# Attention on one core: the eight global keys put into the block of the 96 neighbouring keys

## The reference

```python
scores = scale * np.matmul(q, k.transpose(0, 1, 3, 2))
is_global = pos[None, :] < int(n_global)          # 8
is_local = (rel >= 0) & (rel < int(n_local))      # 96
dist = np.where(is_global & ~is_local, float(n_local), np.abs(rel))
scores = scores - slopes[:, None, None] * dist    # per head
scores = np.where(is_global | is_local, scores, -1e9)
a = softmax(scores); attn = a @ v
x = moe(attn)      # token mixing, then a 512 -> 1536 -> 512 layer
out = moe2(x)      # angles, cos and sin products, token mixing, a last layer
```

## Time and profile before

| | us |
|---|---|
| median of 3 runs (528.63 to 528.68) | 528.64 |
| the profiled execution's own time | 529.02 |
| its span, first to last instruction | 527.2 |
| steps 8 to 46 of attention, 26.44 to 102.37 | 75.93 |
| first product of the mixing layers starts at | 109.53 |

### The profile page before, as it was taken

The page is one execution under the profiler, slowest core; times in us unless marked ns, Lnnn a source line. Parts: engine busy times, 40 slices in busy tenths (PEclk is TensorE's granted clock), DMA queues, the critical chain, the costliest instruction groups (busy, mean ns, idle before and its releaser), DMA issues.

```text
span 527.2 us, 8284 instructions
## 1 busy us (share of the span) xinstructions
PE 509.6 (97%) x3092; PEld 475.3 (90%) x3092; DVE 267.1 (51%) x671; ACT 181.8 (34%) x466; POOL 139.9 (27%) x129
## 2 busy tenths in 40 slices
PE   2999989999999999999999999999999999999997
PEld 2899889978999999987999999998888899888897
DVE  6888999845211232136211144327775584665452
ACT  4899889842111121113111123532223230331120
POOL 3555545339970000001300004550220130000040
PEclk9999999999999999999999999999999999999999
DMA  7754554403440000000300003140000011000002
GB/s 264 266 180 136 208 178 142 141 2 127 173 137 4 1 1 0 2 0 1 121 0 1 0 1 121 60 140 0 1 1 1 1 62 61 0 1 0 1 31 90
DMA packets 9258, 35.02 MB, mean 66 GB/s; under 512 B 1153, under 2 KB 3201, under 8 KB 7809
## 3 DMA queue, kind: packets, MB, share of 16 engines
q1 hardware_dynamic: 9216, 34.48, 19.1%
HBM read 31.33 MB, written 3.15 MB: 65 GB/s over the span
## 4 chain that ended last, share of the span: by engine, by line
PE 90%; DVE 6%; issue 2%; ACT 1%; DMA 1%; DVEq 0%; ACTq 0%
PE bank L271 70%; PE bank L1338 6%; PE bank L1121 5%; PE bank L1084 4%; PE bank L1102 2%; PE bank L1194 1%; DVE scores L855 1%; PE bank L1221 1%; DVE wsplit L770 1%; DVE wsplit L781 1%; PE bank L1149 1%; ACT probs L625 1%; DMA counts<-both_counts 1%; ACT probsT L579 0%; DVE act_raw L797 0%
## 5 line engine op out<-in xcount | busy, mean ns | idle before, releaser
L271 PE MATMUL bank<-hid,wsplit 128*128 128x384 f32 (+1 forms) x648 | 126.4, 344 | 0.1
L271 PEld LDWEIGHTS bank<-hid,wsplit 128*128 128x128 f32 x648 | 113.3, 188 | 3.9 <-issue 0.7
L271 PE MATMUL bank<-split,wsplit 128*128 128x384 f32 x576 | 108.1, 337 | 0.0
L271 PE MATMUL bank<-wsplit,zs 128*128 128x512 f32 (+1 forms) x576 | 104.1, 340 | 0.0
L271 PEld LDWEIGHTS bank<-wsplit,zs 128*128 128x128 f32 x576 | 89.1, 188 | 13.3
L271 PEld LDWEIGHTS bank<-split,wsplit 128*128 128x128 f32 x576 | 100.3, 188 | 0.0
L990 DVE SCALAR_TENSOR_TENSOR hid<-bank,hid 128x384 fp32r<-128x384 f32 x48 | 26.7, 557 | 140.4 <-ACT hid L704 140.4
L557 POOL TENSOR_TENSOR wsplit<-wraw,wsplit 128x1536 fp32r<-128x1536 f32 (+1 forms) x18 | 58.7, 3261 | 75.3 <-ACT wsplit L665 74.2
L704 ACT ACTIVATE hid<-bank 128x384 fp32r<-128x384 f32 x48 | 23.6, 491 | 143.8 <-PE bank L271 143.8
L556 POOL CAST wsplit<-wraw 128x1536 fp32r<-128x1536 f32 (+1 forms) x12 | 15.9, 1326 | 129.2 <-PE bank L271 123.0
L1084 PE MATMUL bank<-wsplit 128*128 128x232 f32 (+2 forms) x224 | 39.8, 310 | 10.0 <-DVE wsplit L830 9.0
(11 more groups left out here) (103 smaller groups left out, 534.5 us busy)
## 6 DMA issues: line engine op xcount, KB each, us to landing
wraw<-weights SPq DMA_DIRECT2D x16, 768.0 KB, 4.0
qk_raw<-qk SPq DMA_DIRECT2D x11, 1056.0 KB, 5.0
vt<-v SPq DMA_DIRECT2D x12, 256.0 KB, 3.2
out<-act_raw SPq DMA_DIRECT2D x16, 192.0 KB, 1.9
wraw<-weights SPq DMA_DIRECT2D x4, 512.0 KB, 3.5
qk_raw<-qk SPq DMA_DIRECT2D x1, 792.0 KB, 5.6
vg<-v_first SPq DMA_DIRECT2D x2, 256.0 KB, 5.6
qk_raw<-qk SPq DMA_DIRECT2D x1, 264.0 KB, 3.4
```

The costliest lines, as they stand in the source:

```text
L271: mm = pe.matmul(dst, lhs(a), rhs(c), start=first and i == 0, stop=last and i == 2, skip_group_check=True)
```

## The change

The eight global keys are treated as if they were part of the block before: places 32 to 135 of a row of `probs` (the 96 neighbours and the 8 global keys) are 104 keys that stand beside each other, and are turned in one transpose and weighed in one product with a second half of `vt`, in which the host has put the 96 value rows of the block before and the 8 global rows. In units 0 and 6 the block has the 8 global keys alone. The path of `gprobs`, `gprobsT`, `vg` and `o_ready` is gone. The ring of keys has six places, one for each unit of a batch, so no unit wraps.

```diff
-RING = 4
-PROBS_AT = 4
+RING = T
+PROBS_AT = 3
-PT_HEAD = REACH + P
+SEEN = REACH + G
+PT_HEAD = 2 * P
@@ SyncE
-                if n >= 3:
-                    sp.wait_ge(o_ready, n - 1)
-                sp.dma_start(vt[:, n % 3], v[b, t]).then_inc(v_in[n % 3], 16)
-                if t == 0:
-                    if b:
-                        sp.wait_ge(vg_lo, b)
-                    sp.dma_start(vg[:, :], v_first[b]).then_inc(vg_in, 16)
+                if n >= 2:
+                    sp.wait_ge(pv_done, PAIRS * (n - 1))
+                sp.dma_start(vt[:, n % 2], v[b, t]).then_inc(v_in[n % 2], 16)
@@ ScalarE
-                first = 0 if m // PAIRS % T else REACH
-                src = PT_BANK[m % 2][:, 0:2 * PT_HEAD]...[:, :, first:]
-                act.activation(dst, src, ACT.Copy).then_inc(pT_taken, 1)
+                act.activation(probsT[:, m % 2], PT_BANK[m % 2][:, :], ACT.Copy).then_inc(pT_taken, 1)
-                if n >= 1 and p == 2:
-                    global_probsT(n - 1)
+                if g == 2:
+                    act.wait_ge(pv_done, STEPS)
@@ VectorE
-                if p == 1 and n >= 1:
-                    gather(n - 1)
                 if p == 2 and n >= 1:
-                    global_probsT_lo(n - 1)
                     invert_sums(n - 1)
-                if p == 0 and n >= 2:
-                    take_x(n - 2)
-                if p == 1 and n % T == 1:
-                    global_values_lo(n // T)
+                if p == 3 and n >= 1:
+                    take_x(n - 1)
@@ TensorE: head_scores, transpose_probs, weigh_values
-                else:
-                    windows = [(UNSEEN, P, (RING - 1) * KW + G + UNSEEN), (P, WIN, 0)]
+                keys = SEEN if n % T else G
...
+                    pe.transpose(PT_BANK[m % 2][0:keys, at:at + P], probs[:, n % 2, h, OWN - keys:OWN],
+                                 ident[:, :])
+                    mm = pe.transpose(PT_BANK[m % 2][:, at + P:at + 2 * P], probs[:, n % 2, h, OWN:],
+                                      ident[:, :])
...
+                    pe.matmul(O_BANK[n % 2][:, cols], probsT[:, m % 2, at + P:at + 2 * P], vt[:, n % 2, 0, cols], ...)
+                    mm = pe.matmul(O_BANK[n % 2][:, cols], probsT[0:keys, m % 2, at:at + P],
+                                   vt[0:keys, n % 2, 1, cols], start=False, stop=True, ...)
...
+            for i in range(2):
+                for at in range(0, 2 * PT_HEAD, PT_HEAD):
+                    pe.transpose(PT_BANK[i][:, at:at + P], ident[:, :], ident[:, :])
-                if p == 2 and n >= 1:
-                    pe.transpose(O_BANK[n % 2][:, 0:P], gprobs...)
-                if p == 3 and n >= 1:
-                    for i in range(2):
-                        mm = pe.matmul(O_BANK[(n - 1) % 2][:, :], gprobsT[:, :], vg_split[:, i], ...)
```

More of the change, by code:

```diff
@@ L75, with build @@
 PI_IN = 3.1415925
-def build(nc, qk, v, v_first, both_counts, weights, out):
+def build(nc, qk, v, both_counts, weights, out):
     ctx = ExitStack()
@@ L185, in build @@
         qk_in = [sem(f"qk_in{i}") for i in range(2)]
-        v_in = [sem(f"v_in{i}") for i in range(3)]
+        v_in = [sem(f"v_in{i}") for i in range(2)]
         k_hi = sem("k_hi")
@@ L631, in _ @@
                     keys_hi(n + 1, p)
-                if p == 0 and n % T == 1:
-                    global_values_hi(n // T)
             general_act(act, flag)
@@ L1381 @@
     first_keys = np.broadcast_to(kc[:, 0:1, :, :, 0:G], (B, T, D, H, G))
-    v_first = np.zeros((B, 2, H, G, H, D), v.dtype)
-    for h in range(H):
-        v_first[:, :, h, :, h] = v[:, None, h, 0:G]
+    rows = v.transpose(0, 2, 1, 3).reshape(B, T, P, DM)
+    v_rows = np.zeros((B, T, P, 2, DM), v.dtype)
+    v_rows[:, :, :, 0] = rows
+    v_rows[:, 0, 0:G, 1] = rows[:, 0, 0:G]
+    v_rows[:, 1:, 0:REACH, 1] = rows[:, :-1, UNSEEN:]
+    v_rows[:, 1:, REACH:SEEN, 1] = rows[:, 0:1, 0:G]
     def tiles(w):
```

136 lines of the change are left out of this document (31 added, 105 removed).

## The result

| us | before | after |
|---|---|---|
| median of the runs | 528.64 | 601.98 (four runs, 597.53 to 604.36) |
| the profiled execution's own time | 529.02 | 601.67 |
| its span | 527.2 | 599.9 |
| scores of an ordinary step, start to start | 0.53 | 0.98 |
| a step of an ordinary unit, start to start | 1.6 to 2.1 | 3.39 |

The ratio is 1.138, with a 95% interval of 1.132 to 1.144. The forecast was 522.3 in a range of 517.8 to 527.6: wrong in size and in sign.

What follows compares the result with a forecast made beforehand. TensorE bound attention at 7.14 us a unit, ScalarE within 5%. Start +1.4, steps 8 to 46 -6.7, end -1.0 sum to -6.3 us: 522.7 for the profiled execution, 522.3 as median, range 517.8 to 527.6.

Steps and rivals of the forecast that it cites:

- Part 5, the start: Unit 0 at the low clock gets more expensive: +1.4 us at the scores of step 8, clock rising about 25 us.
- If the clock rises at the same moment: Start: the 3.06 us of added low-rate work is then done after the rise at half price, +1.53.
- the low clock lasts: Rival, attention: 1.5 us per extra low-rate step; 534.2 us if it lasts through units 2 and 3; chance 0.10.
- Part 1, "width doesn't matter": TensorE, ordinary steps: products with values stay 0.70 despite wider weights; step 1.66, unit 6.6 us in place of 7.14.
- No price above a full one: TensorE's products with values over 104 or 8 keys: no price above the 0.09 of a full one.
- Part 2, the wrap: Scores of units 4 and 8 fall from 0.93 to 0.53 a step: 3.2 us of TensorE over 8 steps.
- Part 3, ScalarE: ScalarE loses L596, its copy L579 grows by 0.05; at 1.75 a step it sets the pace over TensorE's 1.66.
- Part 4: Steps 8 to 46: 67.6 us plus 1.6 of stalls, 69.2 in place of 75.93, a gain of 6.7.
- Part 6: End, step 47's scores to first mixing product, 7.16 us before: -1.0, between -0.6 and -1.3.
- Part 7, the loads: Larger vt loads (512 KB a unit), the later second weight and GpSimd's memset change nothing.
- TensorE keeps the pace: Rival, the 39 steps: TensorE's 1.66 a step decides, 64.7 in place of 69.2, time 517.8 us; chance 0.10.

Runs made afterwards that it cites:

- x3: Kernel before with one product of 64 columns in place of the global path's two of 512 once a unit; 527.6 us.
- z1: y1 with 24 added products of 256 columns, result unread, after the scores of step 0; 524.4 us.
- v2: y1 with the block's product for the first 96 queries only, so every second weight load is 96 columns wide; 527.3 us.
- y1: Kernel after with 104 keys in the block product of every unit, units 0 and 6 padded with zeros; 597.0 us.
- z3: Kernel after itself with 24 added products of 256 columns after the scores of step 5; 536.3 us.
- y3: Kernel before with the ring of six places for the keys alone; 526.2 us.
- u3: z1 with the block's product for the first 96 queries only; 523.6 us.
- u1: z1 again, timed in rounds beside the kernel before; 525.16 us, ratio 0.9939.
- v1: u1 with take_x of units 0 to 10 cut to one head of eight, after GpSimd writes zeros to act_raw at the start; 600.7 us.
- x1: Kernel after with 32 added products of 256 columns, result unread, behind the scores of step 0; 601.6 us.
- u2: y3 with z1's 24 added products in step 0; 525.69 us, ratio 0.9941.
- x2: Kernel after with two added products of 512 columns, result unread, in each unit from unit 1 on; 565.8 us.
- y4: Kernel after without the transposes and products of the 8-key block in unit 0 alone; 526.7 us.
- u4: z1 with take_x of unit n-2 at p 1 in place of unit n-1 at p 3; three runs 524.9 to 526.4 us (ratio 0.9927), the fourth 595.0.
- z2: y1 with 24 added products of 256 columns after the scores of step 5; 531.4 us.

## Why the prediction was wrong, point by point

**Part 5, the start, is the step that failed.** "If the clock rises at the same moment" carried the whole sum. It was an assumption about an engine whose load the change raises just there: unit 0 has eight products with values in a step in place of four, and every unit from then on has wider ones. In the kernel after the moment never comes: the scores of step 8 start at 34.41, where 27.8 was forecast, and cost 0.98, and no later step of attention runs at the high rate. And even without the change there was no such moment to count on, as x3 shows: with identical work it lay some 4 us earlier. The 79 us between the forecast and the profiled execution (522.7 and 601.7) are 6.6 ahead of step 8, 65.9 in the 39 steps (135.06 in place of 69.2), 4.9 at the end (11.1 in place of 6.16) and 1.6 in the first mixing products.

**The rival "the low clock lasts"** had the mechanism, the place and the price: 1.5 us a step, and a low step of 3.24, measured 3.39. It was sized wrong by its length (8 steps, where all of attention was meant by its own argument that "each unit from now on has this mix") and by its chance (0.10). I counted against it that the level was held before through steps with waits. That is about holding it, and the rival was about reaching it. With all 48 steps the arithmetic at hand gave some 522 + 40 x 1.5 = 582 us, and such a tail belonged into the range.

**Part 1, "width doesn't matter", is wrong.** I read it from four products at 0.36 against eight at 0.70. But the two first products after other work cost less than the following ones (0.17 against 0.22 in z1's rows), so that a group of four can't be scaled to eight. The direct readings are 0.81 for eight of 128, 0.70 to 0.71 for four of 128 and four of 96. Apart from the chip, this width is the only thing in which v2, whose level rose, differs from y1, whose level didn't; whether it decides that, two single runs don't settle. "No price above a full one" for 8 keys was wrong too: eight products cost 2.30 in unit 0 after the change (24.54 to 26.84), where y1, with 104 keys, has 1.57; at the high rate 1.35 in place of 0.81 (z3).

**Part 2, the wrap, is right** in kind: no scores at 0.93 are left in y3, and unit 4 takes 7.17 in place of 8.76, unit 8 7.85 in place of 8.76. That is 2.5 of the 3.2 forecast, and over the 39 steps 1.9 are left of it; the other 1.2 of y3's 3.1 is the earlier rise.

**Part 3, ScalarE, is right in its numbers**: the copy takes 0.57 to 0.58 (575 ns forecast), the step 1.75 where TensorE is not above it (u3). But that ScalarE would set the pace was wrong: in u1 TensorE, at 1.78, still does.

**Part 4** said 69.2 for the 39 steps. With the level high it is 74.0 in z1 and u1, a gain of 1.9 in place of 6.7, and 75.4 in the kernel after itself (z3, 34.19 to 109.61), whose steps over 8 keys cost 2.33. About 1.4 of the missing 4.8 is TensorE's 0.81 (39 steps at some 1.77 are 69.0, not 67.6), the other 3.4 are waits: 5.0 where I took 1.6 of 2.5. The thought was that VectorE, with three instructions less, would cause fewer. But TensorE's global products, 0.66 a unit, were also the time in which VectorE could catch up, and with the steps as short as the engines allow that cover was gone. This last sentence is argued.

**Part 6** said 6.16 for the end; measured with the level high 6.8, a gain of 0.35 in place of 1.0. **Part 7, the loads,** is right.

The Trainium skill (Perfetto Trace Analysis, section Optimizing Scalar/DVE Operations) says that GpSimd and VectorE share a read port of SBUF. The 4.51 us cast of v1 shows more plainly than the earlier trace rows that the two hold each other up; it stood beside a memset, which has nothing to read, so reading isn't all of it.

The rival "TensorE keeps the pace" was right on who sets the pace of a step without waits in z1 and u1, and wrong on its price. The rule of the Trainium skill named there (Perfetto Trace Analysis, section Identifying the Most-Contended Engine) puts TensorE first in z1 too, with weight loads of 69.64 us in these 73.96 against ScalarE's 69.35; its 517.8 was reached by no run.

**What stays open.** Whether the number of small products, the columns of their weights or something that goes along with both is what keeps the level down. Why x1 lost the level in its fourth step and z1, u1 and u2 with almost the same products didn't; why x2 lost it in unit 6 and y4 and z3 held it there; and how often a run of u1 or u4 would lose it. y1 and v2 are single runs on two chips, if 70 us apart; the kernel after took 597.5 or more in all four of its runs. Why these four lie 6.8 us apart, where those of the kernel before agree to 0.1, no trace shows.

## What to carry to other kernels

Where the trace shows TensorE below its higher level for a while and nothing tells what ended that, the moment of the rise is no constant (x3 had it some 4 us earlier with the same work): a change of what runs before it has to be priced with the case that it never comes, over the full length of the stage. Read the level from prices of a known instruction from start to start (0.53 or 0.98 for the same scores), in every stage. The price of small products went with the width of their weights here (0.81 or 0.70 for eight), and rose for a block of 8 keys, so read both before calling a joined product free. And where TensorE and ScalarE stood within 5% of each other, little came of the work that TensorE was to lose: 1.9 us of the 6.7 forecast.

## What the runs showed of the hardware that I had not expected

- TensorE worked without a gap from 16.07 to 179.7 us (busy 163.63 of 163.63), and stayed at 1.2 GHz, with products that move 64, 128 and 232 columns in turn. Wide products (512 columns) went ahead of the rise, between 183.72 and 185.13. The Trainium skill (TensorE: Matmul & The Clock Gate, section "Part 1: The HAM clock gate") lets the level follow how busy the engine has been; busy in the profile's sense does not bring it up here, and the measurement decides.
- The same instructions, at the same times to 0.01 us up to 20.31, were at the higher level from 21.0 us in one execution (x3) and from about 24.9 in another (the kernel before).
- The view of the granted clock reads 1.00 all through that low stretch. In these runs it reads 0.50 only where the level had been granted before and was taken back (x1, x2, v1).
- A difference of 32 columns in every second weight load (0.2 us of 3.4) stood between 597.0 and 527.3 us (y1 and v2, one run each), and 3.76 us of added products between 597.0 and 531.4 (y1 and z2).
- Products over 8 keys cost more than those over 104 with weights of the same width: at the high rate a row of two, and the full row behind it, 0.36 each from start to start in place of 0.22.
- A cast on VectorE of 0.29 us lasted 4.51 beside a memset of 5.21 on GpSimd.
